# Attention, experts and a last layer on one core: the second batch's keys turned in heads 3 to 7 of tile 1 in place of heads 1 to 5

## The chip, the cores and the metric

The kernel runs on one core of one Trainium2 chip. A core has TensorE (matrix products and transposes, PE in the rows), VectorE (DVE), ScalarE (ACT), GpSimd (POOL) and SyncE (SP, which issues the DMAs here). Each engine runs its own list of instructions in order and waits on semaphores that the others count up. The metric is device time in microseconds (us), the median of several runs.

## What is computed

Three layers in a row. Attention over 2 batches, 8 heads, 576 tokens of 64 values, where each query keeps only its 32 highest scores:

```
scores = scale * np.matmul(q, k.transpose(0, 1, 3, 2))
kth = np.partition(scores, -top_k, axis=-1)[..., -top_k:-top_k + 1]
mask = scores >= kth
scores = np.where(mask, scores, -1000000000.0)
scores = scores - np.max(scores, axis=-1, keepdims=True)
attn = np.exp(scores)
attn = attn / (np.sum(attn, axis=-1, keepdims=True) + 1e-09)
return np.matmul(attn, v).astype(np.float32)
```

Its output, 1152 tokens by 512, goes through eight experts (`h = np.maximum(x @ w1[e], 0.0)`, `ye = h @ w2[e]`, hidden width 1024), summed with gates that eight rounds of row and column normalisation give. A last layer multiplies by w_in (512 by 2048), applies `h * np.tanh(sp)` with `sp` the softplus of h, and multiplies by w_out. All is float32 to the outside; most products are made from a high and a low part of each operand.

## The kernel before

The queries are cut into nine tiles of 128 tokens. Tiles 0 to 3 are of batch 0, tile 4 (MIX) is half of each batch, tiles 5 to 8 are of batch 1. A tile runs over its 8 heads (h = 0 to 7). While a head's scores are sorted, the engines do other work: parts of the previous heads, and from head 5 of tile 1 on the chunks of the first experts (`chunk_at`). The order on every engine is written out by hand, head by head, in one `tile_body` for each engine.

A head goes through the engines so. TensorE makes the scores (L608) into PSUM banks 0 and 1; ScalarE copies them to `s_sb` (L1114, as every plain copy of ScalarE); VectorE finds the 32 highest of 576 by four rounds of MAX8 and MATCH_REPLACE8 (L1487, L1489), two heads interleaved as a pair; ScalarE takes the exponentials (L1149); GpSimd (L1961, L1964) or VectorE (L1483) sets the others to zero; TensorE transposes the result (L618, and L622 for the last 64 columns of two heads at once); ScalarE copies it to `pT` and `p_rest`; TensorE multiplies with the values (L632, L637, in `attend`, for both heads of a pair); ScalarE copies to `o_sb`; and VectorE adds up and inverts the row sums (L1496, L1498). All this runs four heads late: head h of a tile transposes and attends head h - 4, so that tile 1's head 3 ends tile 0's head 7. `s_sb` has four buffers.

VectorE takes a tile's row sums between two steps of its own list: in tile 1, those of tile 0 stand in the first pair, ahead of its last step.

The keys must be turned before scores can be made from them: a batch has 576 keys, 5 chunks (KC = 5), four of 128 rows and one of 64. ScalarE copies a chunk's high part (`keys_high`), VectorE (batch 0) or GpSimd (batch 1, `keys_low`) makes the low part, TensorE turns both together in 2 sets of 4 transposes (`keys_transposed`, L589, one set for each half of the heads), and ScalarE copies each set to `k_s` (`keys_copied`). For batch 1 the sets use PSUM banks 4 and 6 every time, so a chunk's transposes wait until the chunk before is copied. Batch 1's keys are first used in tile 4, but since the banks and the buffers of the parts are shared with the experts, expert 1 (tile 2, head 5) waits for the last of them (KEYS_1).

The queries of a tile are turned in heads 5 and 6 of the tile before it and in its own heads 0 and 1 (L597). The first expert's chunks on tile 1's head 5 and later are L753 (up) and L760 (down); the other experts of this stage are L728 and L741. SyncE loads its weights into the buffers `w_raw` in which raw keys were, once the low parts of both batches are made (`k_low0`, `k_low1`).

The placement which the change touches is in TensorE's and in ScalarE's `tile_body`, both called for tile 1 alone with `keys=True`:

```
if keys and 1 <= h <= KC:
    pe.wait_ge(k_high, KC + h)
    pe.wait_ge(k_low1, h)
```

Of the kernel before, what the change touches and what calls it, by code (L numbers as in the profile page):

```python
# [11 lines left out]
def build(nc, q, k, v, w_gate, w1, w2, w_in, w_out, spill, out):  # L12
# [22 lines left out]
    KC = TB + 1  # L35
# [40 lines left out]
    with ctx:  # L76
# [3 lines left out]
        def sem(name):  # L80
            return ctx.enter_context(nc.semaphore(name))
# [66 lines left out]
        k_high, k_low0, k_low1, k_copied_d = sem("k_high"), sem("k_low0"), sem("k_low1"), sem("k_copied_d")  # L148
# [6 lines left out]
        k_tr, k_copied, q_tr, q_copied = sem("k_tr"), sem("k_copied"), sem("q_tr"), sem("q_copied")  # L155
# [64 lines left out]
        def head(T, h):  # L220

            return T * H + h
# [4 lines left out]
        def chunk_at(T, h):  # L227

            e, f = (T - MIX + 2, h + NF - LAG) if h < LAG else (T - MIX + 3, h - LAG)
            return (None, None) if isinstance(T, int) and e < 0 else (e, f)  # L230

        def new_x(e, f):

            return isinstance(e, int) and e < 3 and f == 0
# [26 lines left out]
        def key_parts(b, c):  # L261

            j = b * KC + c
            n = P if c < TB else REST
            return (w_hi, w_lo)[j // RING % 2][0:n, j % RING, :, :].rearrange("p a n -> p (a n)").rearrange(
                "p (h a d) -> p h a d", h=H, a=2)
# [8 lines left out]
        def key_columns(c, bank):  # L275
# [3 lines left out]
        KEY_BANKS = {(0, 0): (HA_BANK, 6, PT_BANK, O_BANK, HA_BANK), (0, 1): (6, 5, 7, 6, 5),  # L279
                     (1, 0): (HA_BANK,) * KC, (1, 1): (6,) * KC}  # L280
        BY_DVE = (1, 4)
        KEYS_FIRST, KEYS_0, KEYS_1 = KC - 2, 2 * KC - 2, 4 * KC - 2

        def raw_queries(rows=slice(0, P)):
# [295 lines left out]
        def _(pe):  # L580
# [4 lines left out]
            def keys_transposed(b, c, g):  # L585
                n = P if c < TB else REST
                parts = key_parts(b, c).bitcast(F32)
                for i in range(HH):
                    last = nc.tensor.transpose(ps[:, KEY_BANKS[b, g][c], i * P:i * P + n],  # L589
                                               parts[:, g * HH + i, :, :].rearrange("p a d -> p (a d)"),  # L590
                                               ident[0:n, 0:n])
                last.then_inc(k_tr, 1)
# [59 lines left out]
            def tile_body(T, parts, before, has_x=True, keys=False, following=True):  # L652


                early = isinstance(T, int) and T < MIX
                first = isinstance(T, int) and T == 0
                if has_x:
                    pe.wait_ge(x_copied, T - 1)
                for h in range(H):
                    late, late_parts = (T - 1, before) if h < 4 else (T, parts)  # L660
                    expert, f = chunk_at(T, h)
                    if h in (1, 2) and not first:
                        pe.wait_ge(q_copied, 4 * T + h + 2)
                    if h in (6, 7) and following:
                        pe.wait_ge(q_copied, 4 * T + h - 1)
                    if first and h == 4:
                        pe.wait_ge(q_copied, 4)
                        pe.wait_ge(k_copied, KEYS_0)
                    if late_parts is not None:
                        probs_transposed(late, (h - 4) % H)  # L670
                    scores(T, h, parts)
                    if first and 1 <= h < 4:
                        first_keys(h)
                    if expert is not None and not new_x(expert, f):
                        up_a(expert, f)
                    if h in (0, 1) and not first:
                        pe.wait_ge(pt_copied, head(T - 1, h + 4) + 1 + FREE)
                        queries_transposed(T, h + 2)
                    if h in (5, 6) and following:
                        pe.wait_ge(pt_copied, head(T, h - 4) + 1 + FREE)  # L680
                        pe.wait_ge(q_low, T + 1)
                        queries_transposed(T + 1, h - 5)
                    if first and h == 4:
                        pe.wait_ge(v_ones, 2)
                        pe.wait_ge(v_in[0], 16 * V_LOADS)
                    if late_parts is not None:
                        attend(late, (h - 4) % H, late_parts)
                    if not early and h == H - 1:
                        x_transposed(T - 1)
                    if expert is not None:  # L690
                        down_before(expert, f)
                    if expert is not None and new_x(expert, f):
                        up_a(expert, f)
                    if early and before is not None and h == LAG - 1:
                        x_transposed(T - 1)
                    if keys and 1 <= h <= KC:
                        pe.wait_ge(k_high, KC + h)
                        pe.wait_ge(k_low1, h)
                        if h == 1:
                            pe.wait_ge(q_copied, 4)  # L700
                        else:
                            pe.wait_ge(k_copied, KEYS_0 + 2 * h - 2)
                        keys_transposed(1, h - 1, 0)
                        keys_transposed(1, h - 1, 1)

            def first_keys(h):

# [83 lines left out]
            def down_before(e, f):  # L791

                if f > 0:
                    down_a(e, f - 1)
                elif not isinstance(e, int) or e > 0:
                    down_a(e - 1, NF - 1)
# [12 lines left out]
            pe.wait_ge(k_copied, KEYS_FIRST)  # L809
            pe.wait_ge(k_copied_d, len(BY_DVE))  # L810
            tile_body(0, FULL0, None, has_x=False)
# [294 lines left out]
        def _(act):  # L1106
# [16 lines left out]
            def keys_copied(b, c, g):  # L1123
                act.wait_ge(k_tr, KC * g + c + 1 if b == 0 else 2 * KC + 2 * c + g + 1)
                copy(key_place(b, c, g), key_columns(c, KEY_BANKS[b, g][c])).then_inc(k_copied, 1)
# [89 lines left out]
            def tile_body(T, before=True, two_before=True, keys=False, following=True):  # L1215
                early = isinstance(T, int) and T < MIX
                first = isinstance(T, int) and T == 0
                for h in range(H):
                    late, late_on = (T - 1, before) if h < 4 else (T, True)
                    expert, f = chunk_at(T, h)  # L1220
                    if late_on:
                        probs_copied(late, (h - 4) % H)
                    scores_copied(T, h, late_on)
                    if h >= 2:
                        exponentials(T, h - 2)
                    elif before:
                        exponentials(T - 1, H + h - 2)
                    if expert is not None and not new_x(expert, f):
                        hidden_a(expert, f)
                    if h in (0, 1) and not first:  # L1230
                        queries_copied(T, h + 2)
                    if h in (5, 6) and following:
                        queries_copied(T + 1, h - 5)
                    if late_on:
                        output_copied(late, (h - 4) % H, two_before if h < 4 else before)
                    if h == (4 if first else 3) and following:
                        queries_high(T + 1)
                    if not early and h == H - 1:
                        x_copy(T - 1)
                    if expert is not None and new_x(expert, f):  # L1240
                        hidden_a(expert, f)
                    if expert is not None:
                        after_chunk(expert, f)
                    if early and before and h == LAG - 1:
                        x_copy(T - 1, two_before)
                    if first and 1 <= h < 3:
                        keys_copied(0, 2 * h - 2, 1)
                        keys_copied(0, 2 * h - 1, 1)
                    elif first and h == 3:
                        keys_copied(0, 4, 1)  # L1250
                        queries_copied(0, 2)
                        queries_copied(0, 3)
                    elif first and h >= 4:
                        keys_high(1, h - 4)
                    if keys and h == 0:
                        keys_high(1, 4)
                    if keys and 1 <= h <= KC:
                        keys_copied(1, h - 1, 0)
                        keys_copied(1, h - 1, 1)

            queries_high(0)
            keys_high(0, 0)
# [806 lines left out]
```

## Time and profile before

| | us |
|---|---|
| median of 3 runs | 1237.83 (1236.6 to 1238.29) |
| profiled execution | 1236.89 |
| its span | 1235.0 |
| TensorE busy | 1193.1 (97%) |
| VectorE busy | 899.4 (73%) |
| ScalarE busy | 687.7 (56%) |
| GpSimd busy | 642.8 (52%) |
| chain that ended last | TensorE 89%, VectorE 5%, GpSimd 2%, ScalarE 2% |

TensorE is full for nearly all of the span, and the chain that ended last lies on it for 89%. The averages hide the first tenth: there VectorE, which sorts the scores, is the full one, and TensorE waits for it again and again. TensorE's granted clock is full except in a few stretches of that first tenth.

### The profile page before, as it was taken

The numbers are of one execution on the slowest core, as the hardware profiler recorded it, in microseconds if no ns is written. First come the engines' busy times: TensorE is split into PE (matmuls) and PEld (weight loads), VectorE is DVE, ScalarE is ACT, GpSimd is POOL, SyncE is SP. The second block draws the span as 40 slices with busy tenths as digits, with TensorE's granted clock in tenths as the row PEclk, the third lists the DMA queues.
The fourth block names the chain that finished last, engine by engine and source line by source line (L and its number), as shares of the span: only waits on it lengthen the run. The fifth ranks groups of instructions, "written<-read, shape, count | busy, mean of one in ns | idle before, by whom it ended". The sixth has DMA issues, their size and how long they took to land.

```text
span 1235.0 us, 19573 instructions
## 1 busy us (share of the span) xinstructions
PE 1193.1 (97%) x6676; PEld 1067.3 (86%) x6676; DVE 899.4 (73%) x1555; ACT 687.7 (56%) x1227; POOL 642.8 (52%) x393
## 2 busy tenths in 40 slices
PE   4789999999999999999999999999999999999998
PEld 3677889999999998999889889999888888898877
DVE  6999998799999961446646565646464647887876
ACT  5667776767777664442243333333333337888776
POOL 1867866555656568763377666666666631000000
PEclk8789999999999999999999999999999999999999
DMA  9024432323323233332233222222222122222330
GB/s 171 9 88 144 138 103 78 101 88 120 111 77 111 86 113 101 120 103 93 86 106 108 68 86 75 72 80 73 82 67 95 52 69 79 76 69 74 97 127 36
DMA packets 150486, 112.10 MB, mean 91 GB/s; under 512 B 34832, under 2 KB 124944, under 8 KB 150416
## 3 DMA queue, kind: packets, MB, share of 16 engines
q1 hardware_dynamic: 150416, 111.19, 29.8%
q8 instruction: 41, 0.67, 0.2%
q14 instruction: 29, 0.24, 0.1%
HBM read 104.09 MB, written 7.08 MB: 90 GB/s over the span
## 4 chain that ended last, share of the span: by engine, by line
PE 89%; DVE 5%; POOL 2%; ACT 2%; issue 1%; DMA 1%; SPq 0%; DVEq 0%; POOLq 0%; ACTq 0%
PE ps L903 16%; PE ps L728 16%; PE ps L741 15%; PE ps L964 14%; PE ps L1087 7%; PE ps L1031 7%; PE ps L637 4%; PE ps L608 3%; PE ps L618 2%; DVE top L1487 2%; DVE work L1489 2%; PE ps L597 1%; POOL s_sb L1961 1%; POOL e_sb L1964 1%; PE ps L632 1%
## 5 line engine op out<-in xcount | busy, mean ns | idle before, releaser
L1890 POOL TENSOR_TENSOR w_lo<-w_raw,w_hi 128x1024 fp32r<-128x1024 f32 x90 | 219.6, 2440 | 114.3 <-ACT w_hi L1114 114.2
L1114 ACT ACTIVATE w_hi<-w_raw 128x1024 fp32r<-128x1024 f32 (+1 forms) x172 | 179.4, 1044 | 0.6 <-DMA w_raw<-in_k 0.6
L1487 DVE MAX8 top<-work 128x8 f32<-128x576 f32 x216 | 152.2, 746 | 0.0
L728 PE MATMUL ps<-x_hi,w_hi 128*128 128x384 f32 (+3 forms) x384 | 128.2, 334 | 0.1
L728 PE MATMUL ps<-x_hi,w_lo 128*128 128x384 f32 (+3 forms) x384 | 127.4, 332 | 0.0
L728 PE MATMUL ps<-x_lo,w_hi 128*128 128x384 f32 (+3 forms) x384 | 127.2, 331 | 0.0
L1897 POOL TENSOR_TENSOR ha_lo<-h_f,ha_hi 128x384 fp32r<-128x384 f32 (+1 forms) x72 | 72.0, 1000 | 90.5 <-ACT ha_hi L1191 90.5
L903 PE MATMUL ps<-w_hi,h_lo 128*128 128x512 f32 x296 | 117.1, 396 | 0.0
L903 PE MATMUL ps<-w_lo,h_hi 128*128 128x512 f32 x296 | 116.9, 395 | 0.0
L903 PE MATMUL ps<-w_hi,h_hi 128*128 128x512 f32 x296 | 115.3, 390 | 0.0
L1489 DVE MATCH_REPLACE8 work<-top,work 128x576 f32<-128x576 f32 x144 | 105.8, 741 | 0.0
L1639 DVE SCALAR_TENSOR_TENSOR h_lo<-m_r,h_hi 128x384 fp32r<-128x384 f32 x96 | 94.3, 1000 | 14.5 <-ACT h_hi L1348 14.2
L1933 POOL TENSOR_TENSOR w_lo<-w_raw,w_hi 128x1024 fp32r<-128x1024 f32 x24 | 57.8, 2406 | 63.7 <-ACT w_hi L1114 63.7
L1922 POOL TENSOR_TENSOR w_lo<-w_raw,w_hi 128x1024 fp32r<-128x1024 f32 x24 | 57.7, 2406 | 54.2 <-ACT w_hi L1114 54.2
L741 PE MATMUL ps<-w_hi,ha_hi 128*128 128x512 f32 x208 | 85.5, 411 | 0.0
L741 PE MATMUL ps<-w_hi,ha_lo 128*128 128x512 f32 x208 | 82.0, 394 | 0.0
L741 PE MATMUL ps<-w_lo,ha_hi 128*128 128x512 f32 x208 | 81.5, 392 | 0.0
L1483 DVE SCALAR_TENSOR_TENSOR e_sb<-s_sb,top,e_sb 128x576 f32<-128x576 f32 x53 | 71.5, 1365 | 9.8 <-ACT e_sb L1149 9.5
L728 PEld LDWEIGHTS ps<-x_hi,w_hi 128*128 128x128 f32 x384 | 72.2, 188 | 2.6 <-issue 0.3
L728 PEld LDWEIGHTS ps<-x_lo,w_hi 128*128 128x128 f32 x384 | 72.2, 188 | 2.4 <-issue 0.2
L728 PEld LDWEIGHTS ps<-x_hi,w_lo 128*128 128x128 f32 x384 | 72.2, 188 | 1.3
L637 PE MATMUL ps<-vones,pT 128*128 128x65 f32 (+1 forms) x640 | 72.2, 269 | 0.0
(185 smaller groups left out, 3263.8 us busy)
## 6 DMA issues: line engine op xcount, KB each, us to landing
w_raw<-in_moe_w SPq DMA_DIRECT2D x288, 256.0 KB, 2.9
w_raw<-in_moe_w_in SPq DMA_DIRECT2D x32, 256.0 KB, 2.8
w_raw<-in_moe_w_out SPq DMA_DIRECT2D x32, 256.0 KB, 3.1
spill<-y_out SPq DMA_DIRECT2D x5, 768.0 KB, 3.8
y_in<-spill SPq DMA_DIRECT2D x5, 768.0 KB, 4.3
q_parts<-in_q SPq DMA_DIRECT2D x18, 128.0 KB, 3.3
vones<-in_v SPq DMA_DIRECT2D x8, 256.0 KB, 5.1
out<-acc SPq DMA_DIRECT2D x8, 256.0 KB, 2.7
```

The source lines that it names most:

```text
L637: last = nc.tensor.matmul(ps[r:r + n, O_BANK, O_COL + a * DV:O_COL + (a + 1) * DV], pT[:, a, c, r:r + n], vones[:, b, c, h - 1 + a, :], st ...
L728: last = nc.tensor.matmul(ps[:, bank, 0:w], wt[:, s, 0, c * P:(c + 1) * P], xt[:, c, token:token + w], start=(n == 0), stop=(n == len(term ...
L741: last = nc.tensor.matmul(ps[:, bank + t, 0:DM], ht(t * P), wt[:, s, 1, :], start=(first and n == 0), stop=(final and n == 2))
L903: yield nc.tensor.matmul(ps[:, YB_BANK + t, 0:DM], ht, wt[:, s, 1, :], start=(start and n == 0), stop=(stop and n == 2))
L964: last = nc.tensor.matmul(ps[:, bank, 0:BT], wt[:, c * P:(c + 1) * P], xt[:, c, :], start=(i == 0), stop=(i == len(terms) - 1))
L1031: last = nc.tensor.matmul(ps[:, h2_bank(u), 0:w], wt[:, F % RING, 0, c * P:(c + 1) * P], xt[:, c, token:token + w], start=(n == 0), stop=( ...
L1087: last = nc.tensor.matmul(ps[:, bank, 0:DM], hidden2(ht, F, t * P, P), wt[:, F % RING, 1, :], start=(f == 0 and n == 0), stop=(f == NF2 - ...
L1114: return nc.scalar.activation(dst, src, ACT.Copy)
L1487: last = v_.max(top[:, b, op // 2, :], src)
L1489: last = v_.match_replace(work[:, par, :], top[:, b, op // 2, :], src, LOWEST)
L1639: v_.scalar_tensor_tensor(out=hidden_of(h_lo, p, chunk, half), in0=h, scalar=0.0, in1=hidden_of(h_hi, p, chunk, half), op0=ALU.max, op1=AL ...
L1890: g_.tensor_tensor(w_lo[:, s, :, :].rearrange("p a n -> p (a n)"), w_raw[:, s, :, :].rearrange("p a n -> p (a n)"), w_hi[:, s, :, :].rearr ...
```

## The change

The five chunks of batch 1's keys are turned and copied at the end of heads 3 to 7 of tile 1, where it was heads 1 to 5. The waits are the same ones, and the chunk's number is h - 3 where it was h - 1. Nothing else is different: as many instructions, the same banks.

```diff
+        KEYS_AT = 3
...
-                    if keys and 1 <= h <= KC:
-                        pe.wait_ge(k_high, KC + h)
-                        pe.wait_ge(k_low1, h)
-                        if h == 1:
+                    if keys and KEYS_AT <= h < KEYS_AT + KC:
+                        c = h - KEYS_AT
+                        pe.wait_ge(k_high, KC + c + 1)
+                        pe.wait_ge(k_low1, c + 1)
+                        if c == 0:
                             pe.wait_ge(q_copied, 4)
                         else:
-                            pe.wait_ge(k_copied, KEYS_0 + 2 * h - 2)
-                        keys_transposed(1, h - 1, 0)
-                        keys_transposed(1, h - 1, 1)
+                            pe.wait_ge(k_copied, KEYS_0 + 2 * c)
+                        keys_transposed(1, c, 0)
+                        keys_transposed(1, c, 1)
...
-                    if keys and 1 <= h <= KC:
-                        keys_copied(1, h - 1, 0)
-                        keys_copied(1, h - 1, 1)
+                    if keys and KEYS_AT <= h < KEYS_AT + KC:
+                        keys_copied(1, h - KEYS_AT, 0)
+                        keys_copied(1, h - KEYS_AT, 1)
```

The line numbers of the changed kernel are 1 higher up to L696 and 2 higher behind it. On TensorE, heads 1 to 3 of tile 1, from the values of head 1 on, stand so before (L618 and L622 transpose the probabilities, L608 is the scores, L632 and L637 the values, L589 the keys):

```order
L632 MATMUL ps<-vones,p_rest 128x130
L637 MATMUL ps<-vones,pT 128x65 x8
L589 MATMUL ps<-ident,w_lo 128x128 x8
L618 MATMUL ps<-ident,e_sb 128x128 x4
L608 MATMUL ps<-k_s,q_s 128x288 x4
L589 MATMUL ps<-ident,w_lo 128x128 x8
L618 MATMUL ps<-ident,e_sb 128x128 x4
L622 MATMUL ps<-ident,e_sb 128x128
L608 MATMUL ps<-k_s,q_s 128x288 x4
L632 MATMUL ps<-vones,p_rest 128x130
L637 MATMUL ps<-vones,pT 128x65 x8
L589 MATMUL ps<-ident,w_lo 128x128 x8
```

and in the changed kernel so:

```order
L633 MATMUL ps<-vones,p_rest 128x130
L638 MATMUL ps<-vones,pT 128x65 x8
L619 MATMUL ps<-ident,e_sb 128x128 x4
L609 MATMUL ps<-k_s,q_s 128x288 x4
L619 MATMUL ps<-ident,e_sb 128x128 x4
L623 MATMUL ps<-ident,e_sb 128x128
L609 MATMUL ps<-k_s,q_s 128x288 x4
L633 MATMUL ps<-vones,p_rest 128x130
L638 MATMUL ps<-vones,pT 128x65 x8
L590 MATMUL ps<-ident,w_lo 128x128 x8
```

The keys' transposes behind heads 1 and 2 are gone, and chunk 0's stand behind head 3's values. On TensorE too, heads 6 and 7, from head 6's chunk products (L753 up, L760 down, L597 the next tile's queries) on, stand so before:

```order
L753 MATMUL ps<-x_f,w_raw 128x128 x4
L597 MATMUL ps<-ident,q_parts 128x128 x4
L760 MATMUL ps<-w_raw,h_f 128x512
L618 MATMUL ps<-ident,e_sb 128x128 x4
L622 MATMUL ps<-ident,e_sb 128x128
L608 MATMUL ps<-k_s,q_s 128x288 x4
```

and in the changed kernel so:

```order
L755 MATMUL ps<-x_f,w_raw 128x128 x4
L598 MATMUL ps<-ident,q_parts 128x128 x4
L762 MATMUL ps<-w_raw,h_f 128x512
L590 MATMUL ps<-ident,w_hi 128x128 x8
L619 MATMUL ps<-ident,e_sb 128x128 x4
L623 MATMUL ps<-ident,e_sb 128x128
L609 MATMUL ps<-k_s,q_s 128x288 x4
```

The 8 transposes of chunk 3 now stand between head 6's products and head 7's scores.

## Rows read from the trace of the kernel before

**Rows 1.** Busy times by stretch, in us; then TensorE's granted clock, DMA share and GB/s.

```profile
core 0: us, PE busy (x) PEld busy (x) DVE busy (x) ACT busy (x) POOL busy (x), PEclk, DMA share, GB/s
...
57.20:62.80 5.60, 2.96 (x25) 2.51 (x23) 5.60 (x13) 3.75 (x8) 5.43 (x5) 1.00 0.15 34
...
70.80:74.20 3.40, 1.70 (x14) 1.23 (x12) 3.40 (x8) 3.40 (x8) 2.60 (x2) 1.00 0.46 156
74.20:84.40 10.20, 10.20 (x51) 9.86 (x51) 10.20 (x22) 4.34 (x11) 6.65 (x5) 0.50 0.00 0
84.40:98.00 13.60, 13.44 (x102) 11.43 (x100) 13.60 (x28) 9.48 (x23) 8.22 (x6) 1.00 0.37 118
...
103.30:127.10 23.80, 19.21 (x134) 15.95 (x135) 23.21 (x48) 17.52 (x37) 18.33 (x13) 1.00 0.55 167
127.10:150.00 22.90, 22.87 (x172) 21.67 (x173) 22.90 (x48) 17.71 (x39) 21.32 (x14) 1.00 0.32 96
```

**Rows 2.** The same of the keys' transposes (L589) on TensorE alone.

```profile
57.20:62.80 5.60, 1.95 (x16) 1.00 0.15 34
```

**Rows 3.** Chain of work that ended last: start us, us, what.

```profile
62.81 0.66 PE ps L618 x4
63.46 0.12 PE ps L622
...
64.52 0.46 PE ps L632 x2
64.98 1.75 PE ps L637 x16
...
66.81 0.29 ACT o_sb L1114
```

**Rows 4.** Timeline of VectorE: start us, us, engine, line, operation [idle before it, releaser].

```profile
67.12 0.43 DVE L1496 TENSOR_SCALAR rsum<-o_sb 128x4 f32<-128x4 f32 x1 [0.29 <-ACT o_sb L1114]
```

**Rows 5.** Timeline of tile 0's heads 5 and 6 on TensorE, at the half clock.

```profile
33.77 1.09 PE L618 MATMUL ps<-ident,e_sb 128*128 128x128 f32 x4 [1.17 <-POOL e_sb L1964]
...
34.65 0.42 PE L622 MATMUL ps<-ident,e_sb 128*128 128x128 f32 x1
...
34.73 1.31 PE L608 MATMUL ps<-k_s,q_s 128*128 128x288 f32 x4
...
37.67 0.64 PE L632 MATMUL ps<-vones,p_rest 128*128 128x130 f32 x2
...
38.10 3.52 PE L637 MATMUL ps<-vones,pT 128*128 128x65 f32 x16
```

**Rows 6.** Timeline of tile 1's heads 1 to 7, and VectorE's second step of its last pair.

```profile
57.07 1.04 PE L589 MATMUL ps<-ident,w_lo 128*128 128x128 f32 x8
...
57.71 1.08 ACT L1114 ACTIVATE k_s<-ps 128x512 fp32r<-128x512 f32 x2
...
72.21 0.66 PE L618 MATMUL ps<-ident,e_sb 128*128 128x128 f32 x4 [1.17 <-POOL e_sb L1964]
...
75.25 3.51 PE L637 MATMUL ps<-vones,pT 128*128 128x65 f32 x16
...
80.50 1.11 PE L589 MATMUL ps<-ident,w_hi 64*128 64x64 f32 x8
...
86.10 0.65 PE L618 MATMUL ps<-ident,e_sb 128*128 128x128 f32 x4
...
87.54 0.66 ACT L1114 ACTIVATE s_sb<-ps 128x576 f32<-128x576 f32 x1
...
88.36 0.73 DVE top L1487
```

**Rows 7.** Timeline around the waits of TensorE that follow.

```profile
103.34 0.66 PE L618 MATMUL ps<-ident,e_sb 128*128 128x128 f32 x4 [0.25 <-POOL e_sb L1964]
...
117.71 0.68 PE L728 MATMUL ps<-x_hi,w_hi 128*128 128x256 f32 x1
...
127.13 0.63 PE L618 MATMUL ps<-ident,e_sb 128*128 128x128 f32 x4 [2.14 <-issue]
```

## The prediction

> **What bounds the kernel now.** I read three views, in this order: the busy times by stretch, the chain of work that ended last, and the timeline of each engine around the moved steps.
>
> The stretches [rows 1] show three stages. Up to about 103 us VectorE is full (5.60 of 5.60 us, 10.20 of 10.20, 13.60 of 13.60) while TensorE has room: 2.96 of 5.60 us in 57.2 to 62.8. From 103.3 to 127.1 us both are loaded and neither is full all the time. From 127.1 us on TensorE is full (22.87 of 22.90 us), and it stays so to the end of the program. The moved steps lie between 57 and 94 us, in the first stage. There TensorE and ScalarE time is worth nothing by itself; what counts is whether one of their results reaches VectorE late.
>
> The chain that ended last shows where it does. From GpSimd's mask of head 7 of tile 0, which is done at 62.8 us, it runs through TensorE's transposes of those probabilities, ScalarE's copies, TensorE's product with the values, ScalarE's copy of the result and VectorE's row sums [rows 3]. VectorE stood idle 0.29 us before that row sum [rows 4]. So this chain of 4.3 us (62.81 to 67.12) has no slack: each us added to it is a us in which VectorE does nothing. Later the chain returns to VectorE's top-k and from there, through GpSimd's masks, to TensorE's wait that ends at 103.34 us, and to the last long wait of TensorE, 2.14 us before 127.13 us [rows 7]. GpSimd's queue feeds that one, and it follows from the same masks. A delay of VectorE between 67 and 97 us, where it is full and the masks wait for it, therefore moves the start of the full TensorE stage at 127 us, and with it the end, one for one.
>
> **The change, part by part.**
>
> *Removed from heads 1 and 2 of tile 1.* The 8 transposes of each of two chunks (1.95 us of TensorE in 57.2 to 62.8 us [rows 2]) and their two pairs of copies on ScalarE (1.08 us a pair [rows 6]). TensorE waits behind both chunks anyway, for GpSimd's masks, and VectorE has no idle time there. Nothing on ScalarE behind the copies is what VectorE waits for. Direct gain: 0. The most it could be is the 0.29 us of VectorE's idle time [rows 4], since behind that VectorE is full.
>
> *Kept in heads 3, 4 and 5.* Heads 3 and 4 turn chunks 0 and 1 instead of 2 and 3, of the same size: 0. Head 5 turns chunk 2 (128 rows) where it turned chunk 4 (64 rows). At the half clock the small chunk took 1.11 us [rows 6]. Four large transposes took 1.09 us at that clock [rows 5] and eight about 1.85 (1.04 at the full one [rows 6], times the ratio for four, 1.09 to 0.66 [rows 3, 5], would give 1.72). So +0.6 to +0.8 us of TensorE.
>
> *Added to heads 6 and 7.* One large chunk (1.04 us at the full clock) and the small one, with 1.08 us of copies on ScalarE and somewhat less. They stand ahead of the scores of head 7 and of those of tile 2's head 0. The scores of head 7 are the tight ones: their copy ended at 88.20 us (87.54 + 0.66) and VectorE began on them at 88.36 [rows 6], so the slack is 0.16 us.
>
> *Waits and queues.* The new places ask for the same semaphores, all of them long given. No DMA is moved. SyncE's wait before the first expert's weights is for GpSimd's subtractions, which stay where they are. The turned keys are first wanted at 117.71 us, where the second expert begins [rows 7], and the last chunk, behind head 7, is turned some 20 us before that.
>
> *TensorE's clock.* This is the term that I expect to matter. The granted clock fell from 2.4 to 1.2 GHz at 74.2 us, after a stretch (70.8 to 74.2) in which TensorE was busy 1.70 of 3.40 us, and it came back at 84.4 us [rows 1]. That fall cost nothing, since VectorE stayed full. In the changed kernel the stretch from 57.2 to 62.8 us loses 1.95 of its 2.96 us: 1.01 busy of 5.60, 18%, where the stretch that ended in the fall had 50%. So I take it that the clock now falls there, a few us before or at 62.8 us, just ahead of the chain without slack. That chain at 1.2 GHz, by rows of tile 0 where the clock was 0.5 [rows 5]:
>
> - From the first transpose to the end of the fifth: 33.77 to 35.07 us, 1.30 us; at the full clock 62.81 to 63.58, 0.77 [rows 3]. With the scores the end is at 36.04, 2.27 us; the copies in between take 0.9 us as before. The product can start when both are through: 62.81 + 2.27 = 65.08 us, against 64.52. That is +0.56.
> - The product with the values: 37.67 to 41.62 us, 3.95 us; at the full clock 64.52 to 66.73, 2.21 [rows 3]. That is +1.74.
> - Sum: +2.30 us at VectorE's row sum, all of it idle time of VectorE.
>
> What then comes after? GpSimd's masks and VectorE's pairs are 2.3 us later, so TensorE and ScalarE get 2.3 us more to bring the scores; heads 3 and 4 are dense by now (scores, transposes of x and of keys in a row), so the clock should be back before head 6. Head 7's scores have 0.16 us of slack as before. Work put in front of them: 1.04 us, and up to 0.8 in head 5; against it TensorE no longer runs heads 5 and 6 at half speed, where the full clock saves some 1.7 us on the product with the values alone (3.51 us [rows 6] against 1.75 [rows 3]). I take 0 here. The end moves by **+2.3 us**.
>
> *A rule that speaks against this term.* The Trainium skill ("TensorE: Matmul & The Clock Gate", Part 4: PE-mode transpose) says that transposes don't count as activity of TensorE for the clock in the way that products do. By it, taking away transposes would change no clock, and the sum would be 0 in place of +2.3. The rows here don't favour it. In 57.2 to 62.8 us two thirds of the busy time was transposes of keys [rows 1, 2]. What was left, 1.01 of 5.60 us, was less dense than the 1.70 of 3.40 us ahead of the fall at 74.2 us, and yet the clock stayed at 2.4 GHz.
>
> **The rivals.**
>
> *No change at all (clock untouched, everything hidden).* For it: the rule above, and that the clock held through 57.2 to 62.8 us as it is, with 2.96 of 5.60 us. Against it: 1.01 of 5.60 us is less than half of the share ahead of the fall at 74.2 us. Time: 1237.8 us.
>
> *Crowding at the old clock.* The clock falls at 74 us as before, and head 5's larger chunk (+0.75) and head 6's new one (+1.04) push head 7's scores: 1.8 - 0.16 = 1.65 us of idle time for VectorE at 88.4 us. It needs the half clock up to 84 us. Time: 1237.8 + 1.65 = 1239.5 us.
>
> *Slower: the clock falls early and stays down.* If the half clock lasts from 62 us into head 7, heads 5 to 7 carry their work at half speed with more key transposes in them. Before, TensorE had heads 5 and 6 from 72.21 to 86.10 us [rows 6], 13.9 us, of which 10.2 at the half clock. With the 3.7 us at the full clock doubled, 0.75 for head 5's larger chunk and 1.85 for head 6's new one it would be 20.2 us. They would start at 74.5 us, so head 7 at 94.7. It may start at 88.6 at the latest (86.10, the 0.16 us of slack, and 2.3), so up to 6.1 us come on top of 2.3. It decides from the point where TensorE reaches head 7 later than 88.6 us. For it: before, the clock came back only after 10.2 us of full TensorE [rows 1]. Against it: that stretch was mostly products with few columns (65) and waits for them, and heads 3 and 4 hold scores and transposes in a row. Time: 1237.8 + 2.3 + 4, some 1244 us.
>
> *Faster.* The 0.29 us before the row sum, or TensorE's waits at 98 to 103 us turned to use by a clock that doesn't fall at 74 us. The latter end with GpSimd's masks, not with TensorE. By the trace that is 1237.5 us at best; what would lie more than 0.2% under the median has no place in it, and gets a chance only because a trace is one execution.
>
> **How the numbers follow.** The profiled execution took 1236.89 us (span 1235.0), 0.9 us under the median of the three runs, 1237.83. The sum on the profiled one is 1236.89 + 2.3 = 1239.2; on the median it is 1240.1, and I give 1240.0. A measurement of this kernel can tell about 0.2%, 2.5 us, from no change, so 2.3 us lies just inside "no change".
>
> Chances: early fall with +2.3 us, 0.59 (its own range is +0.9, where the clock is back before the product with the values is over, to +3.3); nothing changes 0.15; crowding 0.08; clock stays down 0.10; faster 0.08. Of the first, two in five parts would measure above +2.5 us: 0.23. With 0.09 from the long half clock and 0.01 from crowding, slower has 0.33. Faster by over 0.2% has 0.05, most of the faster case. The rest, 0.62, is no change. The range from 1237.0 to 1243.5 us leaves out the faster cases, the lower part of "nothing changes" and most of the long half clock, some 2 in 10.
>
> **What would show it.** Right: in the profile after, the granted clock is 0.5 from a point between 58 and 63 us on; VectorE's idle time before the second row sum grows from 0.29 to about 2.6 us; TensorE's wait ending at 103.34 and the one at 127.13 us both come 2.3 us later, and from 127 us on the two traces are the same, shifted. Crowding: the idle time of VectorE appears before the maximum over head 7 of tile 1 instead. Long half clock: both. Nothing changed: the clock is 1.0 through 57 to 70 us. What would make me wrong most easily is the clock, which falls and rises at points that I can only bound from a few stretches.

## The result and the profile after

The changed kernel takes 1239.99 us (median of 20 runs, 1239.21 to 1241.79) against 1238.06 for the kernel before (20 runs, 1236.39 to 1241.6): 1.0017 times, 95% interval 1.0011 to 1.0024. That is a loss of 1.9 us (1.4 to 3.0) that is clear of noise; its middle lies inside the 0.2% that the prediction calls no change, its upper end does not. 1240.0 was forecast. One run of an experiment below, the lengthened chain, took 1983.39 us at a mean clock of 0.555 and counts in none of the ratios. The profiled execution took 1239.42 us with a span of 1237.6, which is 2.6 us over the span before.

The busy times by stretch answer to [rows 1], with the columns of there:

```profile
57.20:62.80 5.60, 1.54 (x9) 1.23 (x10) 5.60 (x13) 2.34 (x5) 5.43 (x5) 0.77 0.12 26
62.80:67.20 4.40, 4.40 (x20) 4.10 (x21) 3.82 (x10) 2.28 (x5) 1.47 (x2) 0.50 0.45 142
67.20:70.80 3.60, 3.60 (x19) 3.33 (x19) 1.37 (x4) 1.71 (x5) 1.09 (x2) 0.54 1.00 291
...
74.20:84.40 10.20, 7.20 (x59) 6.77 (x60) 10.20 (x23) 6.16 (x15) 5.93 (x4) 0.99 0.00 0
84.40:98.00 13.60, 13.44 (x89) 10.83 (x89) 13.28 (x29) 8.96 (x22) 9.00 (x7) 0.88 0.24 79
```

The clock column is the news. It was 1.00 from 57.20 to 74.20 us and is 0.50 in 62.80 to 67.20 now; VectorE, the third busy time, does 1.37 us in a stretch of 3.60. In the kernel before the half clock lay in 74.20 to 84.40 us, where VectorE stayed full. The edges of the fall, by more rows of the same view:

```profile
57.20:60.12 2.92, 0.63 (x6) 0.66 (x7) 2.92 (x8) 0.23 (x1) 2.84 (x3) 1.00 0.22 50
60.12:62.80 2.68, 0.91 (x5) 0.56 (x5) 2.68 (x7) 2.11 (x4) 2.60 (x3) 0.53 0.00 0
...
70.36:84.02 13.66, 9.53 (x79) 8.65 (x77) 13.66 (x29) 9.53 (x22) 9.31 (x7) 1.00 0.13 44
84.02:87.43 3.41, 3.41 (x15) 2.79 (x14) 3.41 (x9) 2.39 (x6) 3.13 (x3) 0.52 0.02 5
```

TensorE was busy 0.63 of 2.92 us at 2.4 GHz, then the clock fell at 60.12 us and stayed at 1.2 GHz until 70.36. The same 2.92 us of the kernel before held 1.38 us of work:

```profile
57.20:60.12 2.92, 1.38 (x14) 1.17 (x12) 2.92 (x7) 1.36 (x3) 2.84 (x3) 1.00 0.26 60
```

The chain of the kernel after, to be laid beside [rows 3]:

```profile
62.63 1.12 PE ps L619 x4
63.75 0.21 PE ps L623
63.96 0.96 PE ps L609 x4
64.92 0.76 PE ps L633 x2
65.68 3.31 PE ps L638 x16
```

It starts 0.18 us earlier than before, and its product with the values takes 4.07 us (0.76 and 3.31) where it took 2.21. The timeline of VectorE, with the answer to [rows 4] on its first line:

```profile
69.40 0.17 DVE L1498 TENSOR_SCALAR rsum<-o_sb 128x4 f32<-128x4 f32 x1 [2.74 <-ACT o_sb L1116]
69.61 0.18 DVE L1500 RECIPROCAL rinv<-rsum 128x4 f32<-128x4 f32 x1
...
90.79 0.76 DVE L1489 MAX8 top<-s_sb 128x8 f32<-128x576 f32 x1 [0.32 <-ACT s_sb L1116]
...
110.31 0.20 DVE L1498 TENSOR_SCALAR rsum<-o_sb 128x4 f32<-128x4 f32 x1 [0.52 <-ACT o_sb L1116]
```

and its counterparts of the kernel before:

```profile
67.58 0.18 DVE L1498 RECIPROCAL rinv<-rsum 128x4 f32<-128x4 f32 x1
...
107.87 0.20 DVE L1496 TENSOR_SCALAR rsum<-o_sb 128x4 f32<-128x4 f32 x1 [0.52 <-ACT o_sb L1114]
```

The idle time before the row sum grew from 0.29 to 2.74 us. The reciprocal behind it is 2.03 us late, less than the row sum (2.28), since the row sum itself is listed with 0.17 us in place of 0.43. (Why is open: it is listed with 0.42 or 0.43 behind 0.28 to 0.30 us of idle time, with 0.16 or 0.17 behind none and behind 0.87 us or more.) The 0.32 us before the maximum over head 7 are new; with them the row at 110.31 us is 2.44 us late. From there to the end of the span it is 1127.29 us, and 1127.13 before (1235.0 - 107.87): what the change costs arises before 110 us. TensorE's last long wait, of [rows 7], shows the same shift, 127.13 to 129.62:

```profile
129.62 0.63 PE L619 MATMUL ps<-ident,e_sb 128*128 128x128 f32 x4 [2.23 <-issue]
```

### The profile page after: what moved, and what is told of

It reads as the page before. It is cut to its first block, busy times and chain, and to the rows that moved or that the text cites. A ratio compares the mean times of both kernels' runs of the same rounds, so it can differ in the third digit from the quotient of the medians.

```text
span 1237.6 us, 19573 instructions
## 1 busy us (share of the span) xinstructions
PE 1194.6 (97%) x6676; PEld 1068.9 (86%) x6676; DVE 899.0 (73%) x1555; ACT 687.5 (56%) x1227; POOL 642.0 (52%) x393
## 4 chain that ended last, share of the span: by engine, by line
PE 90%; DVE 4%; ACT 2%; POOL 2%; issue 1%; DMA 1%; SPq 0%; ACTq 0%; DVEq 0%; POOLq 0%
PE ps L905 16%; PE ps L730 15%; PE ps L743 15%; PE ps L966 14%; PE ps L1089 8%; PE ps L1033 8%; PE ps L638 4%; PE ps L609 3%; PE ps L619 2%; DVE work L1491 2%; DVE top L1489 2%; PE ps L598 1%; POOL s_sb L1963 1%; PE ps L633 1%; DMA q_parts<-in_q 1%
```

## The experiments

The question is whether the thinned TensorE work in heads 1 and 2 causes the loss by way of the clock, or whether the new places do. Most experiments put work that nobody reads on an engine. On TensorE it is this, into a PSUM bank (YA_BANK) that is free then:

```
def filler(n):
    parts = key_parts(1, 0).bitcast(F32)
    for i in range(n):
        nc.tensor.transpose(ps[:, YA_BANK, i % HH * P:i % HH * P + P],
                            parts[:, i % HH, :, :].rearrange("p a d -> p (a d)"), ident[:, :])
```

The kernel before was run again beside each group of experiments, and each ratio is to the runs of its own group: medians of 1238.19 us (33 runs; fillings of heads 1 and 2 together, half of the move, longer chain, more filler in heads 1, 2 and 4), 1237.44 (34 runs; ScalarE's time, removal without heads 6 and 7, filler in both tiles) and 1238.12 (21 runs; head 1 or head 2 alone). The changed kernel was not repeated in them but for one execution, so that an experiment is laid beside it by way of these ratios. For all of them the mechanism is read from one profile each.

In what follows the *tail* is the time from VectorE's row sum at about 108 to 111 us to the span's end.

### TensorE's time in heads 1 and 2 given back

To the changed kernel, at the end of heads 1 and 2 of tile 1:

```
+                    if keys and h in (1, 2):
+                        pe.wait_ge(k_high, KC + 1)
+                        pe.wait_ge(k_low1, 1)
+                        filler(8)
```

> The changed kernel with 8 transposes whose result nobody reads at the end of heads 1 and 2 of tile 1 on TensorE, where the two chunks were; ScalarE gets nothing there. Clock theory: the granted clock stays 1.0 from 57 to 74 us, VectorE's idle time before the second row sum is 0.3 us again (2.74 in the changed kernel). The clock then falls at 74 us as in the kernel before, and the keys of heads 5 and 6 are in the way at the half clock: some 1.6 us of idle time before the maximum over head 7. End: +1.6 us on the kernel before, if that second idle time comes, +0 if it doesn't. Rival, transposes don't hold the clock or the new places alone cost the time: idle time before the row sum stays 2.7 us, end +2.0 us or more.

Measured: 0.9997 of the kernel before (0.9988 to 1.0006), 1237.53 us. This interval and that of the changed kernel (1.0011 to 1.0024) don't meet: 16 transposes that nobody reads win the loss back. Its timeline on TensorE shows the chain at 2.4 GHz again (columns as in [rows 5]):

```profile
61.77 1.04 PE L599 MATMUL ps<-ident,w_lo 128*128 128x128 f32 x8
62.74 0.66 PE L626 MATMUL ps<-ident,e_sb 128*128 128x128 f32 x4
...
64.75 1.90 PE L645 MATMUL ps<-vones,pT 128*128 128x65 f32 x16
```

The first line is filler; the values take 1.90 us, where a row at the half clock has 3.52 [rows 5], and VectorE has no idle time before the row sum. Before the maximum over head 7 it idled 0.28 us, where 1.6 had been expected if the clock fell at 74 us; it fell at 81.4 us and for 3.4 us only, so that the case for the 1.6 us did not come up. The clock was low from 47.27 to 57.51 us in this execution, another place than in the kernel before, at 0.56 us of idle time for VectorE at 58.03. That fall pushed work of head 1 into the stretch ahead of the chain:

```profile
57.51:62.80 5.29, 5.29 (x47) 5.12 (x46) 4.77 (x11) 3.33 (x8) 5.12 (x5) 0.97 0.22 50
```

TensorE was full there with more than the filler. So this profile shows that the chain runs at 2.4 GHz, and not that the filler alone is what kept it so; the medians show that the filler wins the time back.

The same in one head only, `h in (1,)` and `h in (2,)`:

> The changed kernel with 8 unread transposes on TensorE at the end of head 1 alone. The stretch from 57 to 60 us is then as busy as before, the one from 60 to 62.6 us isn't. Clock theory: the fall is prevented in some executions and only put off to 62 to 64 us in the others, where it still meets the chain: between the kernel before and the changed one, +0.5 to +2 us. Rival, one chunk is enough: +0.

> The changed kernel with 8 unread transposes at the end of head 2 alone. The stretch from 57 to 60.7 us stays as empty as in the changed kernel, so the clock falls in most executions ahead of the chain: +1 to +2.3 us. Rival, one chunk is enough: +0.

Measured: 1.0016 (1.0007 to 1.0026) with head 1 filled and 1.0003 (0.9994 to 1.0012) with head 2, the one next to the chain. Against the kernel before, head 1 leaves a loss that can be seen and head 2 none; their own intervals meet, so that head 2 is the better place is likely and not shown. I had expected a loss of head 2 as well, and that was wrong. The profiled execution with head 2 filled had its half clock ahead of the chain, from 55.94 to 62.77 us, and it came back while the filler ran, behind products with values and scores; VectorE idled 0.30 us before the row sum, as in the kernel before:

```profile
62.29 1.33 PE L599 MATMUL ps<-ident,w_lo 128*128 128x128 f32 x8
63.60 0.66 PE L626 MATMUL ps<-ident,e_sb 128*128 128x128 f32 x4
...
65.61 1.90 PE L645 MATMUL ps<-vones,pT 128*128 128x65 f32 x16
```

That with head 1 filled had a like fall, 55.77 to 62.59 us, and idled 0.87 us before the row sum. There it was the work ahead of the chain that ran late:

```profile
66.22 0.46 PE L640 MATMUL ps<-vones,p_rest 128*128 128x130 f32 x2 [0.91 <-ACT p_rest L1127]
```

TensorE waited 0.91 us for ScalarE's copy at the place where it waits 0.42 in the kernel before. In neither of the two profiles did the clock fall in the chain itself, so what tells the two places apart is their medians.

### ScalarE's time given back instead

The removal took work from ScalarE too. In the changed kernel ScalarE makes three copies of 384 columns that nobody reads, in heads 1 and 2:

```
+                    if keys and h in (1, 2):
+                        for unread in (h_f, ha_hi, ha_lo):
+                            copy(unread[:, h - 1, :], ps[:, YA_BANK, 0:BT])
```

> The changed kernel with three unread copies (384 columns each) on ScalarE at the end of heads 1 and 2 of tile 1, where the keys' copies were, and nothing on TensorE. Clock theory: nothing gained on the changed kernel, row sum idle 2.7 us, +2.0 us on the kernel before. Rival, it is ScalarE's work that mattered: back to the kernel before, +0.

Measured: 1.0029 (1.0019 to 1.0038). The loss stays. By stretch:

```profile
57.20:62.80 5.60, 1.22 (x9) 1.03 (x10) 5.60 (x13) 3.89 (x10) 5.43 (x5) 0.87 0.13 29
62.80:67.20 4.40, 4.40 (x20) 4.09 (x20) 3.92 (x10) 3.01 (x7) 1.47 (x2) 0.50 0.41 131
```

ScalarE has its 3.89 us back ([rows 1] has 3.75), TensorE has 1.22, and the clock falls all the same; VectorE idles 2.74 us before the row sum.

### The removal without heads 6 and 7

The changed kernel with chunks 3 and 4 in heads 0 and 1 of tile 2, so that head 7's scores have nothing new ahead of them but head 5's larger chunk (TensorE's part; ScalarE's is changed in the same way):

```
-            tile_body(1, FULL0, FULL0, has_x=False, keys=True)
+            tile_body(1, FULL0, FULL0, has_x=False, keys={3: 0, 4: 1, 5: 2})
...
-            tile_body(2, FULL0, FULL0)
+            tile_body(2, FULL0, FULL0, keys={0: 3, 1: 4})
```

> The changed kernel with chunks 3 and 4 in heads 0 and 1 of tile 2 in place of heads 6 and 7 of tile 1: the removal from heads 1 and 2 alone, without the transposes ahead of head 7's scores. Clock theory: idle time before the second row sum near 2.7 us as in the changed kernel, no idle time before the maximum over head 7 (0.32 us there): end +2.2 us on the kernel before. Rival, crowding in heads 6 and 7 is what costs: end near the kernel before.

Measured: 1.0023 (1.0014 to 1.0033), 1240.71 us. Sparing heads 6 and 7 gives nothing back. The profiled execution is no illustration of the chain: its clock was low from 25.58 to 59.71 us and whole in the chain, and VectorE idled 1.09 us before its row at 48.65 and 0.61 at 59.01 instead. TensorE was late by this fall and therefore busy 5.38 of 5.60 us in 57.20 to 62.80. The verdict rests on the median, and that this median comes from the chain is not seen in a trace.

### Half of the move

`KEYS_AT = 2` in place of 3: the keys in heads 2 to 6.

> Keys in heads 2 to 6: one chunk leaves the stretch from 57.2 to 62.8 us. Clock theory: TensorE is still mostly idle from 57.2 to 60.7 us, so the clock falls there at about 60 us as with both taken away, and the row sum's idle time is near 2.7 us: end +2.3 us. Rival, the cost follows the number of heads moved: half of it, +1.0 us, and a clock of 1.0 until head 3's values are done.

Measured: 1.0005 (0.9996 to 1.0015), 1238.89 us, 0.7 us above the kernel before. I had expected the full 2.3 us, and that was wrong: the interval, -0.5 to +1.9 us, leaves it out. It holds the rival's +1.0 us and 0 as well, so that the cost follows how much is moved fits and is not shown. The profiled execution had its half clock ahead of the chain, 55.61 to 62.44 us, not in it, and VectorE idled 0.90 us before the row sum. Together with head 2's filler it suggests that the work in head 2, right ahead of the chain, matters most; both have TensorE work there and a time near that of the kernel before.

### The chain lengthened by a known length

The kernel before with 16 unread transposes between head 3's scores and its product with the values, no other work touched:

```
                     scores(T, h, parts)
+                    if keys and h == 3:
+                        filler(16)
```

> The kernel before with 16 unread transposes between head 3's scores and the product with head 7's values in tile 1, in the chain to the second row sum, at the full clock. They take 2.08 us, of which 0.42 us lie in a wait for ScalarE. If each us of that chain reaches the end: idle time before the row sum 0.29 + 1.66 = 1.95 us, and the end +1.7 us. Rival, a later slack takes it up: the idle time is there, the end +0 to +0.5 us.

Measured: 1.001 (1.0 to 1.0019), 1239.41 us against 1238.19. The chain:

```profile
64.42 1.75 PE ps L598 x16
66.17 0.23 PE ps L639 x2
66.39 1.75 PE ps L644 x16
...
68.22 0.29 ACT o_sb L1123
...
68.53 0.18 DVE rsum L1505
```

The row sum comes 1.41 us later than in the kernel before, behind 1.62 us of idle time (1.95 expected). The reciprocal behind it starts at 68.74 us, 1.16 later (67.58 before), since the row sum is again listed with 0.17 us. VectorE's row at 107.87 is at 109.02, 1.15 us later, the span's end 1.2, and the median 1.2 (the interval allows 0 to 2.4). So what delay is left behind the row sum goes on to the end whole; no later slack takes it up. This execution had a half clock of its own from about 54.7 to 61.5 us, in heads 1 and 2, in which the kernel is the one before.

### The clock held up

The kernel before with 8 more unread transposes behind the keys of heads 1, 2 and 4:

```
                         keys_transposed(1, h - 1, 1)
+                    if keys and h in (1, 2, 4):
+                        pe.wait_ge(k_high, KC + 1)
+                        pe.wait_ge(k_low1, 1)
+                        filler(8)
```

> The kernel before with 8 transposes whose result nobody reads behind the keys of heads 1 and 2 and behind those of head 4 of tile 1, each in a wait of TensorE. Clock theory: the clock stays 1.0 from 44 us on, in every execution; VectorE's idle time before the row sum stays 0.3 us. TensorE is early in heads 5 to 7, which is worth nothing. Time 0 to 1 us under the kernel before: its median of 20 runs is 1238.06 with runs up to 1241.6, and the slower ones would be those in which the clock fell earlier. Rival: the added transposes delay the transposes of the probabilities behind them, +0.5 us or more.

Measured: 1.0006 (0.9995 to 1.0017), 1239.0 us, and not the lower median I had expected. The profiled execution did what was meant:

```profile
44.46:107.00 62.54, 51.19 (x395) 44.51 (x395) 61.90 (x132) 42.26 (x97) 43.22 (x30) 1.00 0.27 85
```

2.4 GHz for 62 us, and a time of 1236.57 us. Four of its eleven runs had a mean clock of 0.989 and took 1236.57 to 1237.33 us; the other seven had 0.982 to 0.986 and took 1238.20 to 1242.88. They have no trace. Behind 107 us the clock of the profiled execution was low once more, for 3.4 us near 1040 us, as in most of the profiles here, at no cost that can be seen (last section).

With 40 unread transposes (here of `key_parts(0, 3)`) ahead of tile 0's head 4, and 8 each at the end of its heads 4 to 7 and of heads 0, 1, 2 and 4 of tile 1, both placements were run, before and after:

```
                         pe.wait_ge(k_copied, KEYS_0)
+                        filler(40)
...
+                    if first and h in (4, 5, 6, 7) or keys and h in (0, 1, 2, 4):
+                        filler(8)
```

> The kernel before with unread transposes on TensorE in its waits of the first stage: 40 ahead of head 4 of tile 0, 8 at the end of heads 4 to 7 of tile 0 and of heads 0, 1, 2 and 4 of tile 1. Clock theory: 1.0 from about 20 us on in nearly every execution, VectorE's idle times at 47.8 and 67.1 us 0 to 0.3 us, every run near the fastest of the kernel before: median 1236.5 us against 1238.2, a ratio of 0.9987. Rival: the spread of the kernel before has another cause, then the median stays at 1238; or the transposes delay the probabilities behind them, then VectorE's idle times grow and the end is later than before.

> The changed kernel with the unread transposes of the held kernel (40 ahead of head 4 of tile 0, 8 at the end of heads 4 to 7 of tile 0 and of heads 0, 1, 2 and 4 of tile 1). If the clock is the whole cause, the new places are free once it is held: the same time as the kernel before with the same transposes, near 1236.6 us, and no idle time of VectorE at head 7 of tile 1. Rival, the new places cost by themselves: 0.5 us or more over that one.

Measured: old places 1.0013 (1.0001 to 1.0025), 1239.31 us, a loss where a gain to 0.9987 had been expected; new places 1.0008 (0.9999 to 1.0018), 1238.44 us, where 1236.6 had been. Neither holds the clock in every execution: the profiled one of the old places shows it low in four stretches between 20 and 135 us, two of them (to 43.8 us, and 81.36 to 88.19) ahead of 1.67 us of VectorE's idle time at 49.23 us and 0.68 at 90.53. A high mean clock is no gain by itself either: all runs of both had 0.988 or more, those of the kernel before 0.979 to 0.990, and they were no faster. Within one kernel, though, the time goes with it: old places 1236.12 to 1237.91 us in the four runs at 0.994 or above, 1239.07 to 1243.31 in the other eight. The profile of the new places shows 2.4 GHz from 29.06 to 80.26 us:

```profile
66.54 0.43 DVE L1508 TENSOR_SCALAR rsum<-o_sb 128x4 f32<-128x4 f32 x1 [0.28 <-ACT o_sb L1126]
...
88.14 0.76 DVE L1499 MAX8 top<-s_sb 128x8 f32<-128x576 f32 x1 [0.27 <-ACT s_sb L1126]
```

Without the fall the idle time before the row sum is what it was, head 7's scores cost 0.27 us, and the span of 1234.6 us is a little under that of the kernel before. The new places are not slower in themselves as far as this pair can tell. As a faster kernel it is no use: none of these beats the kernel before.

### Both kernels once more

> The changed kernel once more, for a second profile of it. If the fall of the clock between 58 and 63 us belongs to the kernel and not to one execution, it is there again at another moment, and the idle time before the second row sum is over 1 us again. Rival: it was chance, and the idle time is 0.3 us.

> The kernel before once more. The clock doesn't fall between 57 and 63 us, and the idle time before the second row sum is 0.3 us; another fall of the clock, at another place, would show what spreads its runs from 1236.4 to 1241.6 us.

The changed kernel took 1241.64 us, the kernel before 1236.84. VectorE's longest idle times of the changed one:

```profile
48.97 0.76 DVE L1489 MAX8 top<-s_sb 128x8 f32<-128x576 f32 x1 [1.11 <-ACT s_sb L1116]
70.71 0.17 DVE L1498 TENSOR_SCALAR rsum<-o_sb 128x4 f32<-128x4 f32 x1 [2.73 <-ACT o_sb L1116]
```

The 2.73 us are there again, with a half clock from 60.09 to 73.74 us; the 1.11 us come with another fall, 29.37 to 49.85 (in the first profiles of both kernels it ended near 43 us, and 0.24 us were idle there). In this execution the clock stayed at 2.4 GHz from 73.74 us past head 7, and VectorE had no idle time before the maximum over head 7. The row that answers to 107.87 us is at 111.20, and the tail is 1128.6 us, 1.5 over the usual, for a reason told in the last section. The kernel before idled 0.30 us before the row sum, with the clock low in 80.43 to 83.84 us and not in the chain.

## Why the prediction held

**The removal is worth nothing directly.** Right as far as it goes: in the changed kernel nothing came back, and ScalarE's time won nothing when it was given back.

**The clock.** Right in place, in mechanism and in size. It fell at 60.12 us (58 to 63 forecast). The product with the values began 2.28 us behind the chain's start (2.27 in the sum) and took 4.07 us (3.95). The chain started 0.18 us earlier, and the row sum came 2.28 us late against 2.30. That the missing TensorE work and not another part of the move does it rests on three medians: TensorE's filler wins the time back, ScalarE's doesn't, and the removal without heads 6 and 7 keeps the loss. That it works by way of the clock is read from profiles: all three that have neither keys nor filler in heads 1 and 2 and a half clock in the chain (two of the changed kernel, one with ScalarE's filler) have 2.73 or 2.74 us before the row sum. Of those with the full clock in the chain, the lengthened chain apart, eight have 0.30 us or less and two, with a fall just ahead of the chain, 0.87 and 0.90. Among the eight is the removal without heads 6 and 7, which has no keys and no filler in heads 1 and 2 either. The runs without a trace can't show it.

The rule weighed against this term, the Trainium skill's "TensorE: Matmul & The Clock Gate", Part 4: PE-mode transpose, would have the transposes not count for the clock. The runs go against it for transposes as this kernel issues them: 16 of them, unread, moved the time from 1.0017 to 0.9997. That the clock rose while they ran, in the profile with head 2 filled, says less, since products ran just ahead of them.

**One for one to the end.** Nearly. The tails are 1127.13 and 1127.29 us; the measured stretch of the chain by 1.41 us gave 1.15 to 1.2, all that was left behind the row sum. Of TensorE's waits, the one at 127.13 us ended 2.49 us late (2.3 forecast). The other is gone: the transposes of 103.34 us stand at 105.78, 2.44 late, with no wait ahead of them, since TensorE itself was late there.

**Head 7's slack, taken as 0.** Too small, by little. The clock fell a second time, 84.02 to 87.43 us, and head 7 of tile 1 began, behind chunk 3, at 88.63 us where [rows 6] has 86.10:

```profile
87.76 1.04 PE L590 MATMUL ps<-ident,w_hi 128*128 128x128 f32 x8
88.63 0.60 PE L619 MATMUL ps<-ident,e_sb 128*128 128x128 f32 x4
```

That is 2.53 us later, while VectorE was 2.03 later, and it waited 0.32 us. Crowding, held for a rival at 1.65 us, is a companion of 0.3, and a second fall belongs to it: the profiles that have 0.24 to 0.33 us there (changed kernel, keys in heads 2 to 6, and three with filler on TensorE) all have a half clock for 3.4 us somewhere in 80 to 88 us, and the three with the new places and no fall there (the second of the changed kernel, ScalarE's filler, and head 2 filled) have no idle time at head 7. With the old places a fall from 80.43 to 83.84 us cost nothing there, and a longer one, 81.36 to 88.19, stood ahead of 0.68 us. The full 1.65 us, for which the half clock had to last from 74 to 84 us with the new places, came up in no profile. The other rivals fell: the clock did move, and it was back at 70.36 us, long before head 7. Against the long half clock the prediction had held that the stretch from 74.2 to 84.4 us was mostly products with 65 columns and waits for them. It was not: these products are 3.51 us of it, and TensorE was busy 10.20 of 10.20 us.

**The time.** On the profiled pair the loss is 2.53 us (1239.42 - 1236.89), on the medians 1.93. The sum went by one execution of the kernel before, in which no fall behind 20 us cost VectorE more than 0.24 us. Its fastest run took 1236.39 us and the changed kernel's 1239.21, 2.8 apart. That some runs of the kernel before lose time to falls of their own and pull its median up is likely and not shown: both of its traces are of short executions (1236.89 and 1236.84 us). The 2.3 us was a fair size for the mechanism and too large by 0.4 for the medians. That 1240.0 met 1239.99 is luck: the term was 0.4 too large, the median of three runs which it started from 0.2 under that of twenty, and 0.1 went in rounding.

**Open.** Why filler in head 2 does better than filler in head 1 is not settled. Nor is what decides a fall: the share of busy time ahead of it doesn't by itself. In the second profile of the changed kernel TensorE was busy 2.14 of 3.42 us (56.67 to 60.09) ahead of the fall at 60.09 us, a larger share than the 2.96 of 5.60 us at which the clock held in the kernel before [rows 1], and had then been idle since 58.81. Why the two kernels with the old places and more filler are not faster in the median is not settled either; falls at other places, as in the one profile of the second, are a likely cause that the other runs can't show.

## What to carry to other kernels

Where an engine without slack waits for a short chain on TensorE, the TensorE work ahead of that chain is not free to move even if nobody waits for it: it can keep the granted clock up, and here 2 us of removed work made VectorE 2.3 us late in the profile and cost 1.9 us in the median. Before moving work out of a sparse stretch, read the clock column and what TensorE did ahead of each fall, and ask what runs until it comes back. Compare medians of many runs: a profile shows one pattern of falls, and the next execution may have another.

## What was not expected of the hardware

**The falls move from execution to execution of the same kernel.** The kernel before had its half clock from 74.20 to 84.40 us in one profile and from 80.43 to 83.84 in another:

```profile
80.43:83.84 3.41, 2.87 (x13) 2.90 (x14) 3.41 (x8) 1.34 (x3) 3.33 (x3) 0.56 0.00 0
```

The changed kernel's began at 60.12 and 60.09 us, and ended at 70.36 and 73.74. A fall that lasts to 49.85 us, which one of the two profiles of the changed kernel shows, stands ahead of 1.11 us of idle time at VectorE's row at 48.97. Such falls are likely a part of the spread of the kernel before, 5 us; none of its longer runs has a trace.

**A short fall in the full stage costs too.** Five profiles, of filler or changed kernels, have one of 3.4 us between 127 and 136 us, where TensorE has hardly any idle time behind its last long wait. The one with ScalarE's filler:

```profile
129.18:132.59 3.41, 3.41 (x18) 3.41 (x19) 3.41 (x8) 2.23 (x5) 2.90 (x2) 0.56 0.11 38
```

Their tails are 1128.4 to 1128.75 us, against 1126.9 to 1127.4 in the others: 1 to 1.8 us for half the clock over 3.4 us. It begins between 0.4 us before and 1.3 us behind the end of TensorE's last long wait ([rows 7], 2.14 us), in which the engine stands still. The like fall near 1040 us costs nothing to be seen: the tails with it alone are 1126.94 to 1127.43 us, and the two without either fall 1127.05 and 1127.13.
